# Strassen feed-forward kernel: the first block product's operand kept in the dead tile of X, its result copied once, and operand splits moved ahead of the last softplus

## What is computed

```
attn:  k_p, v_p = mean over groups of 8 of the 576 positions      (4 batches, 8 heads, head dim 64)
       attn_out = softmax(q @ k_p^T / 8) @ v_p                    -> x of 2304 tokens x 512
moe:   h = x @ w_in (512 x 2048);  g = h if h >= 1, 0 if h <= -1, else (h+1)^2/4
       x = g @ w_out (2048 x 512)
moe2:  h = x @ w_in2;  g = max(h, 0) + log1p(exp(-|h|));  out = g @ w_out2
```

## Time and profile before

| | |
|---|---|
| runs | 866.34, 867.46, 874.46 us |
| profiled execution | 862.46 us, span 860.7 us |
| TensorE (PE) busy | 845.8 us, 98% of the span |
| DVE, ACT, POOL busy | 592.0, 490.5, 360.8 us |
| h of layer 1 | from 468.4 to 668.5 us of the span, 48 half pairs |
| the 21 product steps of layer 1 | from 669.0 us to the end |

### The profile page before, as it was taken

How to read it: one execution, slowest core, us unless ns; L and a number is a source line. 1 busy time by engine, 2 the same in 40 slices (tenths; PEclk the granted TensorE clock), 3 DMA queues, 4 the chain that set the end, 5 groups by cost and what they waited for, 6 DMA issues and landing times.

```text
span 860.7 us, 13035 instructions
## 1 busy us (share of the span) xinstructions
PE 845.8 (98%) x5198; PEld 822.7 (96%) x5198; DVE 592.0 (69%) x618; ACT 490.5 (57%) x700; POOL 360.8 (42%) x290
## 2 busy tenths in 40 slices
PE   8989999999999999999999999999999899999998
PEld 7768999999999999999999999999999899999998
DVE  4983855532233598768657698898899989778642
ACT  3875665644445453444435868978887654445442
POOL 6994677744454600000000498888766500000000
PEclk9979999999999999999999999999999999999999
DMA  8952767565555896454633235675655698645532
GB/s 195 209 126 78 209 209 230 185 220 188 181 183 188 274 395 224 167 220 154 227 109 99 96 123 189 211 243 182 211 200 176 204 397 306 239 164 203 200 113 73
DMA packets 106539, 167.82 MB, mean 195 GB/s; under 512 B 21872, under 2 KB 94448, under 8 KB 101872
## 3 DMA queue, kind: packets, MB, share of 16 engines
q1 hardware_dynamic: 93800, 157.86, 54.9%
q10 hardware_dynamic: 12680, 9.14, 3.7%
HBM read 96.21 MB, written 70.78 MB: 194 GB/s over the span
## 4 chain that ended last, share of the span: by engine, by line
PE 84%; DVE 6%; ACT 3%; DMA 3%; SPq 1%; issue 1%; POOL 1%; ACTq 0%; DVEq 0%
PE ps L1263 41%; PE ps L1281 37%; DVE t_a L1052 2%; DMA ops<-gops 2%; PE ps L1178 1%; DVE ops L1064 1%; PE ps L1215 1%; DMA w_raw<-in_moe_w_in_dram 1%; PE ps L1296 1%; PE ps L1321 1%; PE ps L1199 1%; DVE xs L992 1%; ACT qT L652 1%; PE ps L1155 1%; DVE t_a L1055 1%
## 5 line engine op out<-in xcount | busy, mean ns | idle before, releaser
L1263 PE MATMUL ps<-xs,W 128*128 128x384 f32 x2304 | 408.2, 336 | 0.8 <-DVE ops L1044 0.8
L1263 PEld LDWEIGHTS ps<-xs,W 128*128 128x128 f32 x2304 | 399.3, 188 | 5.8 <-issue 4.9
L1281 PE MATMUL ps<-xs,Tm 128*128 128x384 f32 x1968 | 345.9, 336 | 3.4 <-DVE xs L992 3.0
L1281 PEld LDWEIGHTS ps<-xs,Tm 128*128 128x128 f32 x1968 | 342.2, 189 | 4.3 <-issue 3.5
L744 ACT ACTIVATE xs<-ops 128x768 fp32r<-128x768 f32 (+1 forms) x148 | 111.7, 826 | 159.1 <-PE ps L1281 149.9
L608 POOL TENSOR_TENSOR ops<-ops 128x384 f32<-128x384 f32 x48 | 72.9, 1519 | 303.2 <-DVE ops L1064 221.9
L992 DVE TENSOR_TENSOR xs<-ops,xs 128x768 fp32r<-128x768 f32 (+1 forms) x148 | 130.2, 941 | 1.8 <-ACT xs L744 1.8
L1044 DVE SCALAR_TENSOR_TENSOR ops<-ps,t_a 128x768 f32<-128x768 f32 x48 | 45.9, 956 | 110.4 <-ACT t_a L768 110.2
L766 ACT ACTIVATE t_a<-ps 128x768 f32<-128x768 f32 x48 | 39.0, 812 | 96.2 <-PE ps L1263 96.2
L1077 DVE TENSOR_TENSOR X<-ps,X 128x768 f32<-128x768 f32 x41 | 38.7, 955 | 77.8 <-PE ps L1281 77.8
L1064 DVE TENSOR_TENSOR ops<-t_a,t_b 128x768 f32<-128x768 f32 x48 | 62.8, 1308 | 19.7 <-ACT t_b L787 17.9
(11 more groups left out here) (88 smaller groups left out, 650.6 us busy)
## 6 DMA issues: line engine op xcount, KB each, us to landing
gops<-ops SPq DMA_DIRECT2D x48, 1344.0 KB, 5.8
ops<-gops SPq DMA_DIRECT2D x36, 1536.0 KB, 6.8
X<-gops SPq DMA_DIRECT2D x22, 384.0 KB, 6.4
w_raw<-in_moe_w_in_dram SPq DMA_DIRECT2D x32, 256.0 KB, 3.9
t_raw<-in_moe_w_out_dram SPq DMA_DIRECT2D x6, 1024.0 KB, 10.0
out_dram<-y_out ACTq DMA_DIRECT2D x11, 384.0 KB, 2.6
k_raw<-in_k_dram SPq DMA_DIRECT2D x10, 288.0 KB
q_raw<-in_q_dram SPq DMA_DIRECT2D x20, 144.0 KB, 7.6
```

Of the source, the lines that this page charges most:

```text
L1263: last = mm(banks[:, tb, :], W[:, slot, f, part, c * P:(c + 1) * P], x[:, x_part, at:at + TB], start=c == 0 and s == 0, stop=c == KC - 1 a ...
L1281: last = mm(banks[:, d, :], Tm[:, t, part, j, d * P:(d + 1) * P], g[:, g_part, at * TB:(at + 1) * TB], start=at == 0 and s == 0, stop=at = ...
```

## The change

1. The even half pair's result is written by two DVE instructions of 384 columns instead of one of 768: G11 goes straight into the dead tile of X, at the place where the first product's fill reads it, G21 into the slot. Odd half pairs stay one instruction. This holds for total (layer 1) and smaller (layer 0).
2. G11 is no longer stored: gops has six operands, stores shrink from 1344 to 1152 KB, and the 22 DMAs gops to X and their semaphores are gone. POOL's sums read G11 from X.
3. Product 0's result is copied into one block of X instead of two; product 1 is added to that copy into the other.
4. Order in layer 1: all four splits of fill 1 stand after half pair 45 (before: two at 45, two at 46). Three of the four splits of fill 2, and the copy of step 0's result, stand ahead of half pair 47's ln (ACT) and of its softplus (DVE).
5. The load for step 3 stands ahead of quad 22's store instead of quad 23's, in both layers.

```diff
-G_PAIR = ((G11, G21), (G12, G22))
-Y_OPS = (((0, 0, None), (0, 1, None)), ((0, 0, (0, 0)),), ((0, 1, (0, 1)),), ((1, 0, (0, 1)),),
+Y_OPS = (((0, 1, None),), ((0, 0, (0, 1)),), ((0, 1, (0, 1)),), ((1, 0, (0, 1)),),
...
+        def first_operand(k):
+            return X[:, k % JJ // 2, TT * (k // JJ) + TB * (k % 2):TT * (k // JJ) + TB * (k % 2 + 1)]
...
-                sp.dma_start(gops[layer][:, i, :, k % JJ, :].rearrange("a p t -> p a t"), ops[:, slot_of(u), 0:PRODUCTS, :]
+                sp.dma_start(gops[layer][:, i, :, k % JJ, :].rearrange("a p t -> p a t"), ops[:, slot_of(u), G12:PRODUCTS, :]
...
-                    if k == QUADS - 1:
+                    if k == QUADS - 2:
                         load_ops(layer, NT)
                     store_ops(layer, k)
-                    if k % JJ >= 2 and k % 2 == 0:
-                        load_first(layer, k // JJ, (k % JJ) // 2 - 1)
-                    if k >= JJ and k % JJ == 0:
-                        load_first(layer, k // JJ - 1, PIECES - 1)
...
                 elif k >= NT:
-                    act.wait_ge(first_loaded[piece], 16 * firsts_until(layer, k - NT, piece))
+                    act.wait_ge(g_made, layer * HPAIRS + 2 * ((k - NT) * JJ + 2 * piece + 1) + 1)
...                                            (ACT, layer 1)
                             if a == HPAIRS - 2:
-                                for piece in range(PIECES // 2):
-                                    fill_hi_piece(fill_of(1, NT + 1), piece)
+                                log(a - 1)
                             exp_abs(a)
-                            if 0 < a < HPAIRS - 1:
+                            if a > 0 and a != HPAIRS - 2:
                                 log(a - 1)
                             plus_one(a)
-                            if a == HPAIRS - 2:
-                                for piece in range(PIECES // 2, PIECES):
+                            if a == HPAIRS - 3:
+                                for piece in range(PIECES):
                                     fill_hi_piece(fill_of(1, NT + 1), piece)
-                                log(a)
...
                 if layer == 1:
+                    for piece in range(PIECES - 1):
+                        fill_hi_piece(fill_of(1, NT + 2), piece)
                     log(HPAIRS - 1)
...                                            (DVE)
             def g_of(n):
-                one, two = G_PAIR[a % 2]
-                return u, ops[:, slot_of(u), one:two + 1:two - one, :]
+                if a % 2 == 0:
+                    return u, [(0, first_operand(a // 2)), (1, ops[:, slot_of(u), G21, :])]
+                return u, [(slice(0, 2), ops[:, slot_of(u), G12:G22 + 1:G22 - G12, :])]
...                                            (total; smaller alike)
-                nc.vector.tensor_tensor(g, t_a[:, a % 2, :, :], t_b[:, a % 2, :, :], ALU.add).then_inc(g_made, 1)
+                for tb, to in g:
+                    last = nc.vector.tensor_tensor(to, t_a[:, a % 2, tb, :], t_b[:, a % 2, tb, :], ALU.add)
+                last.then_inc(g_made, 1)
...
                         else:
+                            if a == HPAIRS - 1:
+                                add_y(1, 0)
+                                for piece in range(PIECES - 1):
+                                    fill_lo_piece(fill_of(1, NT + 2), piece)
                             softplus(a)
                             if a == HPAIRS - 3:
-                                for piece in range(PIECES // 2):
+                                for piece in range(PIECES):
                                     fill_lo_piece(fill_of(1, NT + 1), piece)
                             total(a)
-                            if a == HPAIRS - 2:
-                                for piece in range(PIECES // 2, PIECES):
-                                    fill_lo_piece(fill_of(1, NT + 1), piece)
```

More of the change, by code:

```diff
@@ L187, in pT_of @@
             return pT[:, u % 2, h, :] if u < FIRST else pT_one[:, h, :]
-        gops = [nc.dram_tensor(f"gops{i}", (PRODUCTS, NT, P, JJ, TB), F32).ap() for i in range(2)]
+        gops = [nc.dram_tensor(f"gops{i}", (PRODUCTS - 1, NT, P, JJ, TB), F32).ap() for i in range(2)]
         ps = ctx.enter_context(nc.psum_tensor("ps", [P, 8, BANK], F32))
@@ L354, in build, with x_part, xs_part @@
         turn_number = {m: t for t, m in enumerate(v_of_turn)}
-        LAST_FIRST = NT + NT - 1
-        def x_parts(n, piece):
+        def first_operand(k):
+            return X[:, k % JJ // 2, TT * (k // JJ) + TB * (k % 2):TT * (k // JJ) + TB * (k % 2 + 1)]
+        def x_part(n, piece):
             layer, k = divmod(n, LAYER_FILLS)
[L361 to L364, removed]
             if k < 2 * NT:
-                return [(slice(at, at + PIECE), X[:, piece, TT * (k % NT):TT * (k % NT + 1)])]
+                return X[:, piece, TT * (k % NT):TT * (k % NT + 1)]
             u = use_of(layer, QUADS + k - 2 * NT)
-            return [(slice(at, at + PIECE), ops[:, slot_of(u), 2 * piece:2 * piece + 2, :].rearrange("p j t -> p (j t)"))]
+            return ops[:, slot_of(u), 2 * piece:2 * piece + 2, :].rearrange("p j t -> p (j t)")
+        def xs_part(n, part, piece):
+            return xs[n % 2][:, part, piece * PIECE:(piece + 1) * PIECE]
         b11 = w_raw[:, :, :, :].rearrange("p a f (j d) -> p (a f j) d", d=DH)
@@ L465, in load_ops @@
                 sp.wait_ge(*slot_free(u))
[L466 to L477, removed]
+                sp.dma_start(ops[:, slot_of(u), :, :], gops[layer][p - 1, i, :, :, :]).then_inc(ops_loaded[slot_of(u)], 16)
             for u in range(3):
@@ L609, in s_sums @@
                                         ).then_inc(s_added, 1)
-                nc.gpsimd.tensor_tensor(ops[:, slot, S3, :], ops[:, slot, G11, :], ops[:, slot, G21, :], ALU.subtract
+                nc.gpsimd.tensor_tensor(ops[:, slot, S3, :], first_operand(k), ops[:, slot, G21, :], ALU.subtract
                                         ).then_inc(s_added, 1)
@@ L614, in s_sums @@
                 pool.wait_ge(s_added, 4 * n + 1)
-                nc.gpsimd.tensor_tensor(ops[:, slot, S2, :], ops[:, slot, S1, :], ops[:, slot, G11, :], ALU.subtract
+                nc.gpsimd.tensor_tensor(ops[:, slot, S2, :], ops[:, slot, S1, :], first_operand(k), ALU.subtract
                                         ).then_inc(s_added, 1)
@@ L742, in fill_hi_piece @@
                     act.wait_ge(x_stored, PAIRS * (k + 1) + piece + 1)
-                for data, source in x_parts(n, piece):
-                    last = nc.scalar.activation(xs[n % 2][:, 0, data], source, ACT.Copy)
-                last.then_inc(fill_hi, 1)
+                nc.scalar.activation(xs_part(n, 0, piece), x_part(n, piece), ACT.Copy).then_inc(fill_hi, 1)
             def hi_w(layer, k):
@@ L874, in _ @@
                     if layer < m < STEPS:
-                        for piece in range(PIECES):
+                        for piece in range(PIECES - 1 if layer == 1 and m == 2 else 0, PIECES):
                             fill_hi_piece(fill_of(layer, NT + m), piece)
@@ L990, in fill_lo_piece @@
                 dve.wait_ge(fill_hi, PIECES * n + piece + 1)
-                for data, source in x_parts(n, piece):
-                    last = nc.vector.tensor_tensor(xs[n % 2][:, 1, data], source, xs[n % 2][:, 0, data].bitcast(F32),
-                                                   ALU.subtract)
-                last.then_inc(fill_lo_dve, 1)
+                nc.vector.tensor_tensor(xs_part(n, 1, piece), x_part(n, piece), xs_part(n, 0, piece).bitcast(F32),
+                                        ALU.subtract).then_inc(fill_lo_dve, 1)
             def t_sums(layer, m):
@@ L1043, in smaller @@
                 dve.wait_ge(*slot_free(u))
-                nc.vector.scalar_tensor_tensor(out=g, in0=bank_pair(v_of_pair[a]), scalar=1.0, in1=t_a[:, a % 2, :, :],
-                                               op0=ALU.max, op1=ALU.min).then_inc(g_made, 1)
+                for tb, to in g:
+                    last = nc.vector.scalar_tensor_tensor(out=to, in0=bank_pair(v_of_pair[a])[:, tb, :], scalar=1.0,
+                                                          in1=t_a[:, a % 2, tb, :], op0=ALU.max, op1=ALU.min)
+                last.then_inc(g_made, 1)
             def softplus(a):
@@ L1123, in _ @@
                             add_half(d)
-                    elif m >= 2:
+                    elif m >= (2 if layer == 0 else 3):
                         add_y(layer, m - 2)
                     if layer < m < STEPS:
-                        for piece in range(PIECES):
+                        for piece in range(PIECES - 1 if layer == 1 and m == 2 else 0, PIECES):
                             fill_lo_piece(fill_of(layer, NT + m), piece)
```

8 lines of the change are left out of this document (1 added, 7 removed).

## The result

In alternating executions the kernel before took 866.6 us and the changed one 875.1 (medians of 20 each); the ratio is **1.0094, 95% interval 1.0077 to 1.0112: slower by 0.9%**. The forecast was 879, with 866 to 885 as its range. Each has executions in a slower state (891.46 and 897.33 the slowest), which the medians contain and the ratio leaves out.

What follows compares the result with a forecast made beforehand. PE, busy 98%, bounds the kernel; layer 1's DVE and ACT loop barely keeps up. 13.0 + 0.1 - 1.5 = 11.6 takes the profiled 862.46 to 874.1; with the median 5.0 above, 879 us, range 866 to 885.

Steps and rivals of the forecast that it cites:

- The likeliest case: Layer 1's h: POOL gets turns between the halves of even totals, step 0 starts 13.0 us later; 879 us, chance 0.53.
- The main term: Layer 1's h: halved even totals put +13.0 us on total(43) and with it on step 0; bounds 0 and 17.9.
- rival C: Layer 1's h: halves meet POOL in only part of the quads, the conflict costs half, +6.5; 872.5 us, chance 0.12.
- The transition: Layer 1's change from h to products: of 5.5 us lost, 1.5 come back; the wait moves to fill 4.
- rival D: PE's pauses ahead of step 0 and in h bring its clock down, 1.8 us each fall; 883 us, chance 0.08.
- layer 0's: Layer 0: PE's one wait for the first split instruction grows by 0.1 us, nothing elsewhere.
- A: Layer 1's h: POOL is not let in between halves, a total costs 0.1 us more; 866 us, chance 0.22.

## Why the prediction held, and which sizes were off

**Sign and mechanism: shown.** The likeliest case came: halves, POOL between them, DVE and ACT too slow to make good what quads with splits cost, PE waiting for s late in h and ahead of step 0. The two control experiments (even and odd halves) tell it from a fixed cost per instruction. The Trainium skill (SBUF — State Buffer, Who interferes with whom) says that a VectorE instruction with two SBUF inputs contends with a GpSimd instruction that reads SBUF, and, of the shared pair of ports, that whoever issues first has it for the whole instruction. The trace agrees, for a width that no row of before had: the second half takes 1.38, where two free halves take 1.03 together.

**The main term, +13.0, measured +8.2.** Odd totals in the changed kernel, DVE's timeline (half pairs 9, 17, 21, 23, 25, 35, 43):

```profile
522.11 1.50 DVE L1041 TENSOR_TENSOR ops<-t_a,t_b 128x768 f32<-128x768 f32 x1
...
555.20 0.96 DVE L1041 TENSOR_TENSOR ops<-t_a,t_b 128x768 f32<-128x768 f32 x1
...
572.02 1.51 DVE L1041 TENSOR_TENSOR ops<-t_a,t_b 128x768 f32<-128x768 f32 x1
...
580.71 1.51 DVE L1041 TENSOR_TENSOR ops<-t_a,t_b 128x768 f32<-128x768 f32 x1
...
589.40 1.50 DVE L1041 TENSOR_TENSOR ops<-t_a,t_b 128x768 f32<-128x768 f32 x1
...
630.61 0.96 DVE L1041 TENSOR_TENSOR ops<-t_a,t_b 128x768 f32<-128x768 f32 x1
...
669.79 0.96 DVE L1041 TENSOR_TENSOR ops<-t_a,t_b 128x768 f32<-128x768 f32 x1 [0.74 <-ACT t_b L762]
```

Against the same totals of before (9 at 522.03, 17 at 552.64, 25 at 586.18, 35 at 625.25, 43 at 662.16), each counted from its own H:

| stretch | forecast | measured |
|---|---|---|
| up to total(9) | 0 | +0.7 |
| to total(17) | +4.2 | +2.5 |
| to total(25) | +1.2 | +0.7 |
| to total(35) | +4.2 | +2.1 |
| to total(43) | +3.4 | +2.3 |
| sum | +13.0 | +8.2 |

This term is the step of the forecast that was mis-sized: 4.8 us too much. Several sizes were wrong, nearly all the same way. A plain quad costs 0.8 to 0.9 more, not 1.05: the even total takes 1.86 from start to end, not the 1.94 that I drew. A quad with a POOL split loses nothing where I put +0.3: from total to total it is 580.71 - 572.02 = 8.69, against 8.77 before. POOL comes to its split later and so holds the odd total 1.51 instead of 2.38, which repays the even total's delay. And I miscounted: a split that holds an odd total lengthens the stretch behind that total's start, so five of the thirteen stretches between total(9) and total(35) have one and eight are plain, not nine. Eight times 0.86, less 0.3 for the five, less 1.3 us by which two late stretches of the kernel before were longer than its other plain ones (7.55 and 8.27 instead of 7.3, most of it a wait for PE), is 5.3, the sum of the three middle rows. At the end three quads with a DVE split cost 0.75 to 0.78 each, not 0.85, and the one with the weight copies nothing (10.16 against 10.17). The measured 8.2 is nearer to my rival C (+6.5) than to the forecast, but C's reason isn't what happened: POOL didn't meet the halves in only part of the quads. In 22 of the 24 even half pairs the second half took 1.36 to 1.38.

**The transition, -1.5, measured -0.7.** Step by step, from S (SP's and ACT's timeline of the changed kernel, against the earlier trace rows):

```profile
702.74 0.36 SPq L455 DMA_DIRECT2D gops<-ops  x1
...
712.20 3.05 ACT L720 ACTIVATE xs<-ops 128x768 fp32r<-128x768 f32 x4 [12.40 <-DMA ops<-gops]
```

Store at S + 26.2 (forecast 25.5), data at S + 35.6 (35.1), step 4 at S + 37.6 (36.8). Step 2 without a wait, as forecast; step 3 waits 0.2 instead of 1.3. Small misses in time, and the waits are as drawn; but the kernel with even halves and nothing else got 0.9 back too, so as a gain of the new order the term isn't shown. What I did not see is that this order is the poorer one: I worked out where the 4.1 us of delay to the last store came from and didn't ask what the transition would be without it. The answer was 2.9 us better than before. Nor did I ask what the single copy gives in the old order, where it shortens step 2's wait by 0.95.

**The clock (rival D).** The idle ahead of step 0 was 2.96, forecast 2.7. The small pauses in h (0.77 to 1.31) brought no fall, so that part of D didn't come. My price of 1.8 for a fall compared a step standing alone with 8.33; against such a step at full clock (8.56) it is 1.6. In the changed kernel's profiled execution no clock fell; with the same pause it stood at 0.50 in the two other kernels with halved even totals. That differs between executions, and it may be why the medians are 8.5 apart and the two profiled executions 6.9; I haven't separated it from the start-up's spread.

**Chances.** Slower by over 1% had 0.55, within 1% 0.43. The measured 0.94% lies just inside, with an interval that reaches over the line: of the two I gave the smaller chance to the one that came. That 875.1 lies within 4 us of 879 is in part luck, and no proof of the sizes. For the profiled execution the forecast was 874.1 and 869.35 was measured: 4.8 too much in the main term, 0.1 in layer 0's, 0.8 too little in the transition's, and 0.6 from where H fell. The range from 866 to 885 held all of this, and rival C and half of A besides.

## What to carry to other kernels

Where VectorE and GpSimd both read SBUF, don't count instructions by their columns: count the gaps. Cutting one VectorE instruction in two offers GpSimd a turn in the middle, which cost 0.8 to 0.9 us in each plain quad here and 8.2 over the layer, against 0.7 over the layer where GpSimd had no sum to run; an output with a step between two far places keeps it whole. In front of a point where a store feeds a load, work put ahead of the last producer delays the load (3.6 us of it moved the last store by 3.9 here), and an idle queue earlier is the place to start other loads.

## What the runs showed of the hardware

After the pauses of PE that were followed by 1.2 GHz (2.05 us before; 2.18, 2.33, 2.94, 2.97 and 3.54 in the experiments) the low clock cost 1.5 to 2.5 us; in the changed kernel's profiled execution pauses of 2.96 and 3.59 were followed by no fall at all, the windows of 2 us around them showing 1.00. No pause of 1.44 or less at this transition was followed by one. So the same pause in the same place doesn't always cost the same.
